# Token routing of a mixture layer by a threshold search: six rounds instead of seven, the first with 127 thresholds, four rounds with folded counts

## What is computed

```python
x = attention(q, k, v, i_gate, f_gate, o_gate)     # 3072 x 320
logits = x @ w_gate                                # 3072 x 8
for idx in argsort(-logits.flatten()):             # greedy
    tok, e = idx // 8, idx % 8
    if assigned[tok] >= 0 or counts[e] >= 384: continue
    assigned[tok] = e; counts[e] += 1
for e in range(8):
    out[assigned == e] = relu(x[assigned == e] @ w1[e]) @ w2[e]
h = out @ w_in                                     # 320 x 2048
return where(h > 0, h, exp(min(h, 0)) - 1) @ w_out
```

## Time and profile before

| | us |
|---|---|
| median of three runs (886.72 to 888.78) | 888.7 |
| the profiled execution, its own time | 887.74 |
| its span | 886.0 |
| busy PE, PEld, DVE | 790.1, 734.4, 527.8 |
| busy ACT, POOL | 461.4, 421.1 |

### The profile page before, as it was taken

The page is one execution under the profiler, slowest core; times in us unless marked ns, Lnnn a source line. Parts: engine busy times, 40 slices in busy tenths (PEclk is TensorE's granted clock), DMA queues, the critical chain, the costliest instruction groups (busy, mean ns, idle before and its releaser), DMA issues.

```text
span 886.0 us, 19502 instructions
## 1 busy us (share of the span) xinstructions
PE 790.1 (89%) x6470; PEld 734.4 (83%) x6470; DVE 527.8 (60%) x1535; ACT 461.4 (52%) x981; POOL 421.1 (48%) x467
## 2 busy tenths in 40 slices
PE   1999999994249999999999999999999999999994
PEld 1788888883139899989989989998999899899894
DVE  7475666666774864765476476547647655543441
ACT  1444444431231676387277538726763872784573
POOL 6444444443360475085257508525750852474133
PEclk9999999996557999999999999999999999999998
DMA  3978787842241120121212012121201211120000
GB/s 65 143 135 137 130 135 129 138 79 89 88 124 42 45 67 23 58 80 46 65 46 66 31 53 80 43 68 44 67 24 58 80 46 65 46 79 24 0 2 22
DMA packets 138521, 61.12 MB, mean 69 GB/s; under 512 B 104704, under 2 KB 136704, under 8 KB 138432
## 3 DMA queue, kind: packets, MB, share of 16 engines
q1 hardware_dynamic: 136128, 52.13, 27.1%
q0 software_dynamic: 2304, 7.87, 2.8%
HBM read 51.72 MB, written 8.26 MB: 68 GB/s over the span
## 4 chain that ended last, share of the span: by engine, by line
PE 54%; DVE 7%; POOL 5%; issue 4%; ACT 4%; DMA 1%; SPq 1%; ACTq 0%; POOLq 0%; DVEq 0%
PE bank L1503 6%; PE bank L1573 6%; PE bank L1504 5%; PE bank L1507 5%; PE bank L1574 5%; PE bank L1575 5%; PE bank L1463 3%; PE bank L1511 3%; PE bank L1509 3%; PE bank L1547 3%; PE bank L1549 3%; PE bank L1548 3%; DVE cmp L1112 2%; POOL gl_lo L1024 1%; PE bank L1532 1%
## 5 line engine op out<-in xcount | busy, mean ns | idle before, releaser
L1024 POOL TENSOR_TENSOR gl_lo<-unit,gl_hi 128x384 fp32r<-128x384 f32 x128 | 133.8, 1045 | 128.0 <-ACT gl_hi L1405 127.4
L1573 PE MATMUL bank<-Wo_hi,gl_hi 128*128 128x320 f32 x384 | 123.7, 322 | 5.0 <-POOL gl_lo L1024 5.0
L1574 PE MATMUL bank<-Wo_lo,gl_hi 128*128 128x320 f32 x384 | 118.7, 309 | 0.0
L1575 PE MATMUL bank<-Wo_hi,gl_lo 128*128 128x320 f32 x384 | 118.7, 309 | 0.0
L1274 DVE SCALAR_TENSOR_TENSOR unit<-bank,unit 128x384 f32<-128x384 f32 x104 | 57.8, 556 | 94.2 <-ACT bank L1398 93.9
L1373 ACT ACTIVATE hid_hi<-bank 128x384 fp32r<-128x384 f32 x64 | 31.4, 491 | 133.7 <-PE bank L1511 133.7
L1003 POOL DMA_INDIRECT xg<-x_rows,idx x24 | 23.7, 989 | 157.9 <-PE bank L1511 90.4
L1503 PE MATMUL bank<-x_hi,Wi_hi 128*128 128x384 f32 x256 | 92.3, 360 | 2.0 <-DVE unit L1277 0.9
L1390 ACT ACTIVATE unit<-bank 128x384 f32<-128x384 f32 x128 | 62.0, 484 | 51.3 <-PE bank L1511 50.2
L1504 PE MATMUL bank<-x_hi,Wi_lo 128*128 128x384 f32 x256 | 86.2, 337 | 0.0
L1573 PEld LDWEIGHTS bank<-Wo_hi,gl_hi 128*128 128x128 f32 x384 | 72.2, 188 | 6.8 <-POOL gl_lo L1024 6.7
(11 more groups left out here) (244 smaller groups left out, 2122.8 us busy)
## 6 DMA issues: line engine op xcount, KB each, us to landing
stage<-in_moe_w_dram SPq DMA_DIRECT2D x32, 320.0 KB, 2.9
stage<-in_moe_w_dram SPq DMA_DIRECT2D x32, 256.0 KB, 2.6
stage<-in_moe_w_dram SPq DMA_DIRECT2D x96, 64.0 KB, 2.4
q_in<-in_q_dram SPq DMA_DIRECT2D x24, 160.0 KB, 3.2
k_in<-in_k_dram SPq DMA_DIRECT2D x24, 160.0 KB, 3.9
o_in<-in_o_gate_dram SPq DMA_DIRECT2D x24, 160.0 KB, 4.1
v_in<-in_v_dram SPq DMA_DIRECT2D x24, 160.0 KB, 4.1
x_rows<-xt SPq DMA_DIRECT2D x24, 160.0 KB, 1.9
```

The costliest lines, as they stand in the source:

```text
L1024: nc.gpsimd.tensor_tensor(gl_lo[:, b, :], ex[:, b, :], gl_hi[:, b, :].bitcast(F32), ALU.subtract).then_inc(gl_ok, 1)
L1573: nc.tensor.matmul(acc[j][:, 0:DM], gl_hi[:, f % RG, t_], Wo_hi[:, f, :], start=(f == 0), stop=False)
L1574: nc.tensor.matmul(acc[j][:, 0:DM], gl_hi[:, f % RG, t_], Wo_lo[:, f, :], start=False, stop=False)
L1575: ins = nc.tensor.matmul(acc[j][:, 0:DM], gl_lo[:, f % RG, t_], Wo_hi[:, f, :], start=False, stop=(f == NF2 - 1))
```

## The change

The search has six rounds of 127, 31, 31, 31, 31 and 33 thresholds. `choose_start` and `choose_keys` move into the table class and work on a slice of tiles. In the mixer, DVE does them and the first comparison for the batch before, at tiles 3, 4 and 5 of a batch, so that the first search compares only the last six tiles itself. In rounds 2 to 5 (`FOLDED`) the counts of four tiles stand side by side: `count_parts` is 6 matmuls with 32 moving columns, DVE copies the result to SBUF (`round_parts`), and `fold_parts` adds the four parts with 4 matmuls. The second search has the three column conversions in its first round, each in a bank of its own.

```diff
-STEPS = ((1024.0, 31), (32.0, 31), (1.0, 31), (4096.0, 31), (256.0, 15), (16.0, 15), (1.0, 17))
+STEPS = ((1024.0, 127), (32.0, 31), (1.0, 31), (1024.0, 31), (32.0, 31), (1.0, 33))
 HIGH = 3
+FOLDED = (2, 3, 4, 5)
+SIDE = 4
+SLOT = P // SIDE
...
             def body(b, c):
...
+                if peeled(b):
+                    if c == 4:
+                        tables.early_by_vector(dve)
+                    return
+                whole, at = bass.ds(b * NCH - NCH, NCH), b * KEY_STEPS - KEY_STEPS
+                if c == 3:
+                    dve.wait_ge(tables.early, 4)
+                    dve.wait_ge(lg_ok, b * NCH)
+                    tables.choose_start(dve, whole, NCH, at)
+                elif c == 4:
+                    tables.choose_keys(dve, whole, NCH, at)
+                elif c == 5:
+                    tables.first_compare(dve, whole, NCH, at)
...
+    def choose_keys(self, dve, sl, n, at):
+        nc, E, step = self.nc, self.E, self.key_step
+        score = self.score[:, sl, :]
+        dve.wait_ge(step, at + 5)
+        nc.vector.tensor_scalar(self.key_hi[:, sl], self.key[:, sl], LOW_BITS, None, ALU.arith_shift_right).then_inc(step, 1)
+        nc.vector.tensor_scalar(self.key_lo[:, sl], self.key[:, sl], (1 << LOW_BITS) - 1, None, ALU.bitwise_and).then_inc(step, 1)
+        nc.vector.tensor_reduce(self.top[:, sl], score, AX.X, ALU.max).then_inc(step, 1)
+        dve.wait_ge(step, at + 8)
+        nc.vector.tensor_copy(self.hi[:, sl], self.key_hi[:, sl]).then_inc(step, 1)
+        nc.vector.tensor_scalar(self.lo[:, sl], self.key_lo[:, sl], UNIT, None, ALU.mult).then_inc(step, 1)
+        nc.vector.tensor_tensor(self.pick[:, sl, :], score, self.top[:, sl].unsqueeze(2).broadcast_to([P, n, E]),
+                                ALU.is_equal).then_inc(step, 1)
+
+    def first_compare(self, dve, sl, n, at):
+        nc, many = self.nc, STEPS[0][1]
+        dve.wait_ge(self.key_step, at + KEY_STEPS)
+        return nc.vector.scalar_tensor_tensor(
+            out=self.cmp(many)[:, sl, :], in0=self.hi[:, sl].unsqueeze(2).broadcast_to([P, n, many]), scalar=LOWEST,
+            in1=self.ramp1[:, :].unsqueeze(1).broadcast_to([P, n, many]), op0=ALU.subtract, op1=ALU.is_ge)
...
+        def part_of(k, part):
+            if isinstance(k, int) and k == 0:
+                return slice(G - G // B, G), G // B
+            return (slice(0, G), G) if part is None else (slice(part * G // 2, (part + 1) * G // 2), G // 2)
...
+        def compare_first(k, part):
+            ins = tables.first_compare(dve, *part_of(k, part), keys_at(k))
+            if part != 0:
+                ins.then_inc(cmp_ok, 1)
...
+        def round_parts(k, q):
+            dve.wait_ge(parts_pe, k * len(FOLDED) + q - FOLDED[0] + 1)
+            nc.vector.tensor_copy(parts[:], pParts).then_inc(parts_ok, 1)
...
-        choose_rounds(1, range(1, WITH_COLUMNS))
-        for j in range(NJ):
-            q = WITH_COLUMNS + j
-            round_compare(1, q)
-            columns(0, j)
-            round_test(1, q)
-            round_move(1, q)
-        choose_rounds(1, (ROUNDS - 1,))
-        hidden(0, 0)
-        choose_rounds(1, (ROUNDS,))
-        hidden(0, 1)
+        compare_first(1, None)
+        columns(0, 0)
+        round_test(1, 1)
+        columns(0, 1)
+        columns(0, 2)
+        round_move(1, 1)
+        for q in range(2, ROUNDS + 1):
+            round_compare(1, q)
+            finish_round(1, q)
+            if q == 3:
+                hidden(0, 0)
+            elif q == 5:
+                hidden(0, 1)
...
             for f in range(NF2):
-                q, odd = f // 2, f % 2
+                q, odd = f // 2 - 1, f % 2
                 if after == 2:
-                    if f == 0:
+                    if f == 2:
                         choose_keys(c + 1)
-                    elif f == 1:
-                        round_compare(c + 1, 1)
-                    elif q > 1 and not odd:
+                    elif f == 3:
+                        compare_first(c + 1, 0)
+                    elif f == 4:
+                        compare_first(c + 1, 1)
+                    elif q >= 1 and odd:
+                        if q in FOLDED:
+                            round_parts(c + 1, q)
+                        else:
+                            round_test(c + 1, q)
+                    elif q >= 2:
+                        if q - 1 in FOLDED:
+                            round_test(c + 1, q - 1)
                         round_move(c + 1, q - 1)
                         round_compare(c + 1, q)
-                    elif q > 0 and odd:
-                        round_test(c + 1, q)
                 elu(k, f)
...
+        def count_parts(k, q):
+            pe.wait_ge(cmp_ok, k * ROUNDS + q)
+            for i in range(G // SIDE):
+                ins = nc.tensor.matmul(pParts, cmp_w[:, i * P:(i + 1) * P],
+                                       pick[:, i * SIDE:(i + 1) * SIDE, :].rearrange("p g e -> p (g e)"),
+                                       start=(i == 0), stop=(i == G // SIDE - 1))
+            ins.then_inc(parts_pe, 1)
+
+        def fold_parts(k, q):
+            pe.wait_ge(parts_ok, k * len(FOLDED) + q - FOLDED[0] + 1)
+            for i in range(SIDE):
+                ins = nc.tensor.matmul(pR[:, 0:E], fold[:, i, :], parts[:, i * E:(i + 1) * E], start=(i == 0), stop=(i == SIDE - 1))
+            ins.then_inc(count_pe, 1)
...
-        rounds(1, range(1, WITH_COLUMNS))
-        for j in range(NJ):
-            columns(0, j)
-            rounds(1, (WITH_COLUMNS + j,))
+        columns(0, 0)
+        count_takers(1, 1)
+        columns(0, 1)
+        columns(0, 2)
+        count_thresholds(1, 1)
         up(0, 0)
-        rounds(1, (ROUNDS - 1,))
+        one_round(1, 2)
+        one_round(1, 3)
         up(0, 1)
-        rounds(1, (ROUNDS,))
+        for q in range(4, ROUNDS + 1):
+            one_round(1, q)
...
             for f in range(NF2 + LAG):
                 if f < NF2:
                     up2(k, f)
...
+                q = f // 2 - 1
+                routing = after == 2 and f < NF2 and q >= 1
+                if routing and f % 2:
+                    (count_parts if q in FOLDED else count_takers)(c + 1, q)
+                elif routing and q - 1 in FOLDED:
+                    count_thresholds(c + 1, q - 1)
                 if f >= LAG:
                     down2(k, f - LAG)
...
+                if routing and f % 2:
+                    (fold_parts if q in FOLDED else count_thresholds)(c + 1, q)
```

More of the change, by code:

```diff
@@ L668, in __init__ @@
         self.sums = sb("sums", [P, self.NJ + 1])
+        self.best = sb("best", [P, G])
+        self.score = sb("score", [P, G, E])
+        self.top = sb("top", [P, G])
+        self.pick = sb("pick", [P, G, E], BF16)
+        self.key = sb("key", [P, G], I32)
+        self.key_t = sb("key_t", [P, G], I32)
+        self.key_hi = sb("key_hi", [P, G], I32)
+        self.key_lo = sb("key_lo", [P, G], I32)
+        self.hi = sb("hi", [P, G])
+        self.lo = sb("lo", [P, G])
+        self.cmp_w = sb("cmp", [P, G * first_n + 2], BF16)
@@ L691, in by_gpsimd @@
                                 pattern=[[1, P]], channel_multiplier=-1).then_inc(self.first_ok, 1)
+        nc.gpsimd.affine_select(out=self.fold[:], in_=self.fold[:], compare_op=ALU.not_equal, fill=1.0, base=0,
+                                pattern=[[-SLOT, SIDE], [-1, P]], channel_multiplier=1).then_inc(self.first_ok, 1)
     def by_vector(self, dve):
         nc = self.nc
[L695 to L699, removed]
-        nc.vector.tensor_copy(self.down[:], self.down_i[:])
+        dve.wait_ge(self.const, 5)
+        for q, (step, n) in enumerate(STEPS[1:]):
+            low = 0 if q == len(STEPS) - 2 else 1
+            nc.vector.tensor_scalar(self.ramps[:, q, 0:n], self.ramp_i[:, low:low + n],
+                                    step * (1.0 if q + 1 < HIGH else UNIT), None, ALU.mult)
         nc.vector.tensor_copy(self.slots[:], self.slots_i[:])
@@ L867, in experts, with columns_bank @@
     pEx = bank[6][:, 0:CAP]
+    def columns_bank(k, j):
+        return bank[j] if isinstance(k, int) and k == 0 else pX
     pR = bank[7]
@@ L1576, in down2, with one_round @@
             ins.then_inc(down2_pe, 1)
-        def rounds(k, qs):
-            for q in qs:
+        def one_round(k, q):
+            if q in FOLDED:
+                count_parts(k, q)
+                fold_parts(k, q)
+            else:
                 count_takers(k, q)
-                count_thresholds(k, q)
-        rounds(0, range(1, ROUNDS + 1))
+            count_thresholds(k, q)
+        for q in range(1, ROUNDS + 1):
+            one_round(0, q)
         totals(0)
```

171 lines of the change are left out of this document (85 added, 86 removed).

## The result

The changed kernel takes 911.8 us (median of four runs, 908.2 to 915.0) against 888.7 of the kernel before in the same session: ratio 1.026, 95% interval 1.022 to 1.031. It is slower, by 23 us where the sum said 13 (900.7 against 887.7). The sign is the forecast's and the median lies in the stated range of 881 to 914, but above the 893 to 909 that the forecast gave for itself. The profiled execution (908.3 against 886.0 from its first to its last instruction, +22.3; by its own time, 910.0 us, it is 1.8 under the median) shows where the time went.

The account below looks back on a forecast made before the run. PE bounds the experts, the search chain the two lone searches, where the clock is near half. 887.7 - .8 (lone searches) + 13.8 (six experts at +2.3) = 900.7, so 901; stated range 881 to 914, the forecast's own 893 to 909.

Parts of the forecast that it names:

- The new place of the first comparison: Experts, to step 5: DVE's keys and comparison halves, 6.8 us, end late; PE stands 2.0 us per expert (.5 to 3.0).
- The clock falls: Rival, experts: new stalls halve the clock for three quarters of a step, 2.2 us more per expert, 914; chance .12.
- The threshold sums: Experts, folded rounds: test and sum a step later; .3 us for rounds 2 to 4, .9 for round 5 at step 14.
- What a round costs PE: Six experts with a search: six rounds cost PE 4.04 us where 4.9 was paid before, -.9 per expert.
- Second search: Lone second search: 3.3 us first comparison, second comparison starting 10.4 us in; +1.5 us, between 0 and +2.5.
- issued from 249.80 to 250.83: Second search: third gather's old issue time, landing at 253.7, used to put the second comparison near 256.4.
- First search and listing: Lone first search on six tiles, five comparisons for six: -2.3 us (-3.5 to -1); token listing behind it 0.
- such waits I leave as they are: First search: one comparison took 2.19 us where .93 was due; such waits were kept unchanged in the sum.
- Mixer: Mixer: keys and first comparison, 2.7 us per batch, fit DVE's 2 us of idle per tile; cost 0 (0 to 1).

Follow-up runs that it names:

- the busy PE: Changed kernel plus 16 unread matmuls of 288 columns on PE ahead of the count of step 5 in experts with a search: 903.4 us.
- the last pair: Rounds of 63, 63, 31, 31, 31, 33 thresholds with earlier keys and round-5 test, second search's first comparison halved: 883.4 us; the same without folding: 886.5 us.
- leaving the part out: Changed kernel without keys and first comparison beside the mixer; the first search does all 24 tiles itself: 921.0 us.

## Why the prediction was right, and where it was off

- *The new place of the first comparison.* Right in mechanism and place, mis-sized: 2.0 a search forecast, 2.57 measured, 15.4 in all for 12. From the first key to the end of the second half DVE took 9.0 us (546.83 to 555.87) where 6.8 were summed. The term that failed most is the keys: 1.1 reckoned from their lengths in the old place, 2.5 measured, since their cast and `pick` met POOL's piece of step 0, which the prediction had listed (534.18 to 535.47) but weighed against the halves alone. The first half kept its length and held gl_lo up; the second came behind W_lo and grew by 1.0.
- *The clock falls* was a rival, at 2.2 us in each of six experts on top of the sum. It happened in three, at 1.5 us: 4.6 in all. With the busy PE, where the wait is .5, it does not happen. The forecast had left it out of the sum at a chance of .12, and only that rival's price takes the range as far as 914: that 911.8 lies inside owes something to luck.
- *The threshold sums.* 3.0 in all at step 14 for 5.4 forecast; the others waited for nothing, for 1.8.
- *What a round costs PE.* 15.4 + 4.6 + 3.0 = 23.0, and the experts are 18.1 longer: 4.9 are left as what the rounds saved, .8 per expert, for .9 forecast. The agreement is in part chance. That remainder also holds the 3.2 by which gl_lo's waits grew and the 2.1 of waits for old comparisons that went; with these set apart the work of the rounds fell by some 6. The fold itself saves .19 a round by the last pair, for .22 forecast.
- So of the 4.3 us by which the experts missed their forecast, 4.6 are the clock, 3.4 the comparison, .5 the rounds, and -4.2 the threshold sums: errors that partly cancelled.
- *Second search.* The step that failed is "issued from 249.80 to 250.83": the third gather's time was carried over unchanged, though a 3.33 us comparison had been put just ahead of the second gather. The second comparison began 12.4 us in for 10.4 forecast; with those 2.0 the +1.5 is nearly the measured +3.6.
- *First search and listing.* -3.7 for -2.3. The 1.4 lie in "such waits I leave as they are": before, two comparisons were held up by a Wo_lo (2.19 and 2.23 us), now one is (2.35). And the sum ended with the search. What stands behind it moved forward, POOL's pieces did not, and the 2.4 us of their meeting were not looked for.
- *Mixer.* Forecast 0; +1.4 in the profile lies within the spread of profiled mixers, and leaving the part out did not bring it back.

The Trainium skill, "SBUF — State Buffer", section "Who interferes with whom", was weighed for the comparison's halves, and the traces agree with it there: each later instruction waited out the earlier, 2.74 = 1.74 + 1.0. The same section puts a DMA that seems stalled by a DVE instruction down to GpSimd being kept from the port time it needs to generate descriptors, which might have pointed at the gather; it also names `tensor_tensor` as an operation that was not seen to do this. Here a two-input comparison did lengthen the gather, 3.96 us for .95.

## What to carry to other kernels

Where two engines take turns at a resource, cost a moved instruction by what the *other* engine does in that stretch, and follow also the second engine's queue: here the wait appeared as a late comparison (15.4 us) or as a late gl_lo (17.5 more), and only less work (63 thresholds) or another time for the small instructions (keys at step 0) made much of it go. Cut one long instruction into several where another engine issues short ones beside it: four quarters cost .2 us and gave 2.4 back at the gather. A wait of PE can have a price beyond its length: 1.5 us for a fall of the clock after three of six waits of 2.57. And when something is made earlier, look at what follows it and will now meet work that did not come forward with it.

## What was not expected of the hardware

A comparison on DVE lengthened the issue of an indirect DMA on POOL from .95 to 3.96 us, with no data of either touching the other's. The clock fell to half after three of six waits of the same 2.57 us, and stayed full in the experts where PE stood .5 or 1.0 for the comparison; whether it falls after a given wait could not be told from the rows. Sixteen matmuls of no use made the experts 4.1 us shorter.
